# Attention and two MLPs on one core: the sums of the pooled softmax taken earlier on VectorE, and some splitting work moved to GpSimd

## The reference

```python
q_d, k_d, v_d = (a.reshape(B, H, S // 4, 4, D).mean(axis=3) for a in (q, k, v))
out_up = repeat(softmax(q_d @ k_d.T / 8) @ v_d, 4)            # pooled, 144 x 144
out_local = softmax(where(|i - j| < 4, q @ k.T / 8, -1e9)) @ v  # a band of 7
x = (out_up + out_local) laid out as (2304, 512)
x = ((x @ w1) * (x @ w2)) @ w3 @ w_out                        # d_ff 1024
out = silu(x @ w_in) @ w_out2                                 # d_ff 2048
```

## Time and profile before

| | us |
|---|---|
| median of 3 runs (lowest, highest) | 807.54 (807.38, 809.4) |
| the profiled execution | 807.54 |
| its span in the trace | 805.8 |
| PE busy | 790.7 (98%) |
| DVE busy | 597.3 (74%) |
| ACT busy | 347.7 (43%) |
| POOL busy | 267.3 (33%) |

### The profile page before, as it was taken

The page is one execution under the profiler, slowest core; times in us unless marked ns, Lnnn a source line. Parts: engine busy times, 40 slices in busy tenths (PEclk is TensorE's granted clock), DMA queues, the critical chain, the costliest instruction groups (busy, mean ns, idle before and its releaser), DMA issues.

```text
span 805.8 us, 13920 instructions
## 1 busy us (share of the span) xinstructions
PE 790.7 (98%) x5401; PEld 713.1 (88%) x5401; DVE 597.3 (74%) x952; ACT 347.7 (43%) x791; POOL 267.3 (33%) x341
## 2 busy tenths in 40 slices
PE   7999999999999999999999999999999999999998
PEld 6778888899998999999999898898889889888987
DVE  6998995767687676777678676779677679857644
ACT  6878877422344324432354333254223334433321
POOL 7788765422322331332213131113123113212100
PEclk9999999999999999999999999999999999999999
DMA  9857632110111111011121211223231122413102
GB/s 323 267 162 247 203 124 82 53 53 29 51 53 30 50 52 53 28 53 53 29 100 60 96 58 53 78 80 114 69 93 65 53 75 72 142 53 87 45 0 79
DMA packets 23041, 69.84 MB, mean 87 GB/s; under 512 B 2496, under 2 KB 2496, under 8 KB 22976
## 3 DMA queue, kind: packets, MB, share of 16 engines
q1 hardware_dynamic: 22976, 68.95, 26.3%
HBM read 64.23 MB, written 4.72 MB: 86 GB/s over the span
## 4 chain that ended last, share of the span: by engine, by line
PE 87%; DVE 9%; issue 1%; ACT 1%; DMA 1%; POOL 1%; SPq 0%; DVEq 0%; ACTq 0%; POOLq 0%
PE ps L1035 43%; PE ps L1093 25%; PE ps L1064 13%; PE ps L1115 3%; DVE qkd L741 1%; DVE prob L752 1%; DVE low L760 1%; DVE r L810 1%; DVE tr L704 1%; PE ps L1190 1%; DMA vg<-in_vg 1%; DVE lowd L766 1%; DVE w3t L733 1%; DVE x L795 1%; PE ps L1176 1%
## 5 line engine op out<-in xcount | busy, mean ns | idle before, releaser
L1035 PE MATMUL ps<-xb,wa 128*128 128x384 f32 x2016 | 405.2, 338 | 0.5 <-DVE mu L863 0.5
L1035 PEld LDWEIGHTS ps<-xb,wa 128*128 128x128 f32 x2016 | 355.1, 188 | 22.8 <-DVE mu L863 1.5
L380 POOL TENSOR_TENSOR rw<-rw 128x256 f32<-128x256 f32 x192 | 169.0, 901 | 451.0 <-DMA rw<-in_sets 337.6
L863 DVE TENSOR_TENSOR mu<-ps,mu 128x384 f32<-128x384 f32 x132 | 73.2, 555 | 121.2 <-PE ps L1035 120.4
L1064 PE MATMUL ps<-g,r 128*128 128x512 f32 (+1 forms) x576 | 124.9, 338 | 1.9 <-issue 1.9
L604 ACT ACTIVATE a<-a 128x384 f32<-128x384 f32 x72 | 37.9, 526 | 188.3 <-DVE a L863 188.3
L1093 PE MATMUL ps<-w2h_even,g 128*128 128x512 f32 x432 | 113.2, 394 | 0.0
L1093 PE MATMUL ps<-w2h_odd,g 128*128 128x512 f32 x432 | 112.5, 393 | 0.0
L710 DVE TENSOR_TENSOR wa<-rw,wa 128x1024 fp32r<-128x1024 f32 x96 | 106.8, 1113 | 3.6 <-ACT wa L443 3.5
L1064 PEld LDWEIGHTS ps<-g,r 128*128 128x128 f32 x576 | 97.7, 188 | 10.5 <-issue 2.5
L1093 PEld LDWEIGHTS ps<-w2h_odd,g 128*128 128x128 f32 x432 | 79.9, 188 | 11.9
(11 more groups left out here) (79 smaller groups left out, 727.5 us busy)
## 6 DMA issues: line engine op xcount, KB each, us to landing
rw<-in_sets SPq DMA_DIRECT2D x48, 512.0 KB, 3.5
w2r<-in_w_out SPq DMA_DIRECT2D x24, 512.0 KB, 3.5
qk<-in_qk SPq DMA_DIRECT2D x16, 576.0 KB, 6.6
vg<-in_vg SPq DMA_DIRECT2D x16, 336.0 KB, 4.3
vw<-in_vw SPq DMA_DIRECT2D x16, 320.0 KB, 3.2
out<-osb SPq DMA_DIRECT2D x18, 256.0 KB, 2.3
wn<-in_w SPq DMA_DIRECT2D x16, 256.0 KB, 4.5
raw<-in_w_out SPq DMA_DIRECT2D x2, 1024.0 KB, 12.3
```

The source lines that it names most:

```text
L380: nc.gpsimd.tensor_tensor(blocks[:, o, :], blocks[:, a, :], blocks[:, b, :], op).then_inc(done, 1)
L863: nc.vector.tensor_tensor(o, half_bank(k, i), term, ALU.add).then_inc(sum_ready, 1)
L1035: e = nc.tensor.matmul(ps[:, (k + i) % 2, 0:TH], wa[:, k % 2, l, A_SLOT[i], a * P:(a + 1) * P], xb[:, i, r, a, :], start=(i in (0, 1, 4) a ...
```

## The change

It is confined to the attention part:

- DVE: `totals_down(s)`, which stood behind `min_local(s+1)`, now stands behind `w3_low`, ahead of the low parts of `w_out`, of `EXTRA`, and of `mask_local(s+1)` and `min_local(s+1)`. In step 0 `min_local(1)` comes right behind `totals_local(0)`. The low parts of `w_out` move from behind `max_down` to behind `totals_down`.
- `W_OUT` is spread over three steps instead of four (three, three, two blocks), and the middle block of each (1, 4, 7) gets its low part on GpSimd, at the head of its step; there are two semaphores instead of one, and PE waits for the one that belongs to the block.
- ACT: `copy_ptd` moves from ahead of `exps_down` to behind it. The factor 1/4 of the pooled values goes from `take_down` into `totals_down`.
- The sums: 1e-9 is added by a `tensor_scalar` instruction instead of by a reduction over pairs whose second element GpSimd had filled with 1e-9.
- GpSimd: `norm_d` ahead of `shift_local(s+1)` except in step 0, and the second set of weight sums in steps 9 to 12 instead of behind step 15.
- Loads: `qk(1)` is issued by ACT at its start; SP's first ones are qk(0), vg(0), vw(0), qk(2); the first half of `w_out` goes behind qk(3) and vg(2).
- Eight warm-up transposes instead of nine.

```diff
-        W_OUT = {1: (0, 1), 2: (2, 3), 3: (4, 5), 4: (6, 7)}
+        W_OUT = {1: (0, 1, 2), 2: (3, 4, 5), 3: (6, 7)}
+        R3_POOL = [W_OUT[s][1] for s in W_OUT]
...
@@ SP @@
-            for s in range(3):
-                load_qk(s)
-                if s == 1:
-                    load_vg(0)
-                    load_vw(0)
+            load_qk(0)
+            load_vg(0)
+            load_vw(0)
+            load_qk(2)
             for t in range(PAIRS):
                 if t == 1:
-                    load_w_out(0)
                     load_qk(3)
                 if t + 1 < PAIRS:
                     load_vg(t + 1)
+                if t == 1:
+                    load_w_out(0)
...
@@ GpSimd, step @@
+                for n in W_OUT.get(s - 1, ())[1:2]:
+                    pool.wait_ge(r3_hi, n + 1)
+                    nc.gpsimd.tensor_tensor(r3[:, n, 1, :], raw3[:, n, BANK:], r3[:, n, 0, :].bitcast(F32),
+                                            ALU.subtract).then_inc(r3_lo_pool, 1)
                 pool_values()
                 if s == 0:
                     shift_local(0)
-                if SUMS[0] <= s < SUMS[0] + 4:
-                    weight_sum(0, s - SUMS[0])
+                for k in range(2):
+                    if SUMS[k] <= s < SUMS[k] + 4:
+                        weight_sum(k, s - SUMS[k])
                 pool.wait_ge(inv_l, s + 1)
                 nc.gpsimd.tensor_tensor(pr, pr, inv[:, u, :, None].broadcast_to([P, 10, BW]), ALU.mult
                                         ).then_inc(norm_l, 1)
-                if s + 1 < PAIRS:
+                if s == 0:
+                    shift_local(1)
+                pool.wait_ge(inv_d, s + 1)
...
+                if 0 < s < PAIRS - 1:
                     shift_local(s + 1)
-                normalise_down()
...
@@ ACT @@
+            act.dma_start(qk_at(1).rearrange("p c s -> p (c s)"), qk_in[1, :, :]).then_inc(qk_here[1], 16)
...
-                    nc.scalar.activation(od[:, (s - 1) % 2, :], ps[:, pO, 0:SD], ACT.Copy, scale=1.0 / POOL
-                                         ).then_inc(od_ready, 1)
+                    copy_act(od[:, (s - 1) % 2, :], ps[:, pO, 0:SD]).then_inc(od_ready, 1)
...
                 if s > 0:
                     copy_pt()
-                    copy_ptd()
                 if s == 0:
                     act.wait_ge(blank, 2)
                 exps_down()
+                if s > 0:
+                    copy_ptd()
...
@@ DVE @@
-                nc.vector.tensor_reduce(tot1[:, u, :], tot[:, u, :, :], AX.X, ALU.add).then_inc(added_l, 1)
+                nc.vector.tensor_scalar(tot1[:, u, :], tot[:, u, :], 1e-9, None, ALU.add).then_inc(added_l, 1)
...
-                nc.vector.tensor_reduce(totd1[:, u, :], totd[:, u, :, :], AX.X, ALU.add).then_inc(added_d, 1)
+                nc.vector.tensor_scalar(totd1[:, u, :], totd[:, u, :], 1e-9, float(POOL), ALU.add,
+                                        ALU.mult).then_inc(added_d, 1)
...
                 max_down(s)
-                for n in W_OUT.get(s - 1, ()):
-                    dve.wait_ge(r3_hi, n + 1)
-                    nc.vector.tensor_tensor(r3[:, n, 1, :], raw3[:, n, BANK:], r3[:, n, 0, :].bitcast(F32),
-                                            ALU.subtract).then_inc(r3_lo, 1)
                 if s == 0:
                     mask_local(1)
                 elif s + 1 < PAIRS:
                     pool_pair(s + 1)
                 totals_local(s)
+                if s == 0:
+                    min_local(1)
                 for q in splits_of(s):
                     w3_low(q)
+                totals_down(s)
+                for n in W_OUT.get(s - 1, ())[0::2]:
+                    dve.wait_ge(r3_hi, n + 1)
+                    nc.vector.tensor_tensor(r3[:, n, 1, :], raw3[:, n, BANK:], r3[:, n, 0, :].bitcast(F32),
+                                            ALU.subtract).then_inc(r3_lo_dve, 1)
                 if s in EXTRA:
...
                 if 0 < s < PAIRS - 1:
                     mask_local(s + 1)
-                if s < PAIRS - 1:
                     min_local(s + 1)
-                totals_down(s)
...
@@ PE @@
-                    pe.wait_ge(r3_lo, n + 1)
+                    if n in R3_POOL:
+                        pe.wait_ge(r3_lo_pool, R3_POOL.index(n) + 1)
+                    else:
+                        pe.wait_ge(r3_lo_dve, n - sum(m < n for m in R3_POOL) + 1)
...
-            warm(9)
+            warm(8)
```

More of the change, by code:

```diff
@@ L141, in attention_then_mlps @@
         gate = sb("gate", [1, 2])
-        tot = sb("tot", [P, 2, 10, 2])
-        totd = sb("totd", [PD, 2, 4, 2])
+        tot = sb("tot", [P, 2, 10])
+        totd = sb("totd", [PD, 2, 4])
         tot1 = sb("tot1", [P, 2, 10])
@@ L149, in attention_then_mlps @@
         vt = sb("vt", [KC, 3, 2 * D])
-        sb("hold2", [P, 1024 - 80 - 42 - 28 - 6 * D])
+        sb("hold2", [P, 1024 - 80 - 42 - 6 * D])
         ps = ctx.enter_context(nc.psum_tensor("ps", [P, 8, BANK], F32))
@@ L165, in attention_then_mlps @@
         consts = sem("consts")
-        blank, small = sem("blank"), sem("small")
+        blank = sem("blank")
         scored, p_turned, summed_d, summed_l = sem("scored"), sem("p_turned"), sem("summed_d"), sem("summed_l")
@@ L180, in attention_then_mlps @@
             sem("w3_hi"), sem("w3_lo"), sem("w3_mul"), sem("w3o_hi"), sem("w3o_lo"))
-        r3_hi, r3_lo = sem("r3_hi"), sem("r3_lo")
+        r3_hi, r3_lo_dve, r3_lo_pool = sem("r3_hi"), sem("r3_lo_dve"), sem("r3_lo_pool")
         tr_ready, xb_hi, xb_lo = sem("tr_ready"), sem("xb_hi"), [sem(f"xb_lo{n}") for n in range(7)]
@@ L205, in attention_then_mlps @@
         LATE = 3
-        W_OUT = {1: (0, 1), 2: (2, 3), 3: (4, 5), 4: (6, 7)}
+        W_OUT = {1: (0, 1, 2), 2: (3, 4, 5), 3: (6, 7)}
+        R3_POOL = [W_OUT[s][1] for s in W_OUT]
         SUMS = (5, 9)
         HIGHS = (7, 9)
-        EXTRA = {9: ("weights", 0), 10: ("tokens", 0), 11: ("tokens", 1), 12: ("tokens", 2), 13: ("tokens", 3),
-                 14: ("weights", 1)}
         FILL = {1: (30, 4, 2), 2: (6, 6, 2), 3: (6, 6, 2)}
@@ L422, in step @@
                                         ).then_inc(norm_l, 1)
-                if s + 1 < PAIRS:
+                if s == 0:
+                    shift_local(1)
+                pool.wait_ge(inv_d, s + 1)
+                pd = prob_d[:, u, :, :, 0:SD].rearrange("p c h k -> p (c h) k")
+                nc.gpsimd.tensor_tensor(pd, pd, invd[:, u, :, None].broadcast_to([PD, 4, SD]), ALU.mult
+                                        ).then_inc(norm_d, 1)
+                if 0 < s < PAIRS - 1:
                     shift_local(s + 1)
-                normalise_down()
             for s in range(PAIRS):
                 step(s)
-            for i in range(4):
-                weight_sum(1, i)
             pool.wait_ge(xb_hi, 3)
@@ L496, in exps_down @@
                                                      scale=D ** -0.5 / POOL ** 2,
-                                                     accum_out=totd[:, u, 2 * g + h, 0:1])
+                                                     accum_out=totd[:, u, 2 * g + h:2 * g + h + 1])
                     e.then_inc(exp_d, 1)
@@ L505, in exps_local @@
                             e = nc.scalar.activation(pr, pr, ACT.Exp, bias=low[:, u, n:n + 1], scale=-1.0,
-                                                     accum_out=tot[:, u, n, 0:1])
+                                                     accum_out=tot[:, u, n:n + 1])
                     e.then_inc(exp_l, 1)
@@ L772, in totals_local @@
                 dve.wait_ge(exp_s, s + 1)
-                nc.vector.tensor_reduce(tot[:, u, 2 * LATE:10, 0].rearrange("p (g h) -> p g h", h=2),
+                nc.vector.tensor_reduce(tot[:, u, 2 * LATE:10].rearrange("p (g h) -> p g h", h=2),
                                         prob[:, u, LATE:NG, :, :], AX.X, ALU.add).then_inc(sum_l, 1)
@@ L839, in _ @@
             pool_pair(0)
-            dve.wait_ge(small, 2)
             mask_local(0)
```

2 lines of the change are left out of this document (removed).

## The result

| | before | after |
|---|---|---|
| median, us (runs) | 807.46 (4) | 818.75 (4) |
| lowest, highest | 807.34, 809.4 | 818.4, 820.48 |
| profiled execution | 807.54 | 818.61 |
| its span | 805.8 | 816.8 |

The ratio is 1.0139, with a 95% interval of 1.0117 to 1.016: 11.3 us slower, where 8.1 had been forecast (815.6, range 811 to 820). The sign, the mechanism and the range held; the size was 3 us short, and two mis-sized terms partly hid each other.

What follows compares the result with a forecast made beforehand. DVE was taken as full in steps 3 to 5, PE and DVE in later steps. +3.4 us by step 3's start and 4.7 from there to step 15 made +8.1 on 807.5: 815.6 us, range 811 to 820.

Steps and rivals of the forecast that it cites:

- The ring by DVE: Attention steps: DVE waits for ACT's pooled exponentials before the next step's minimum, which ACT awaits; 7.35 + X us per step.
- exp_d(3): End of ACT's exponentials of the pooled scores in step 3 (one pair of heads), forecast at 35.15 us.
- The small instructions behind the wait: Two small DVE instructions after the wait for pooled exponentials, 0.16 each: 0.33 us with the signal.
- X: DVE work placed between `totals_down` and the next mask: 1.0 us in steps 10 to 14, 1.7 per pair of low parts.
- The ring by PE: Attention steps: PE's `weighted_down` waits for the late `copy_ptd`; 7.8 us per step against 7.57.
- The start: Loads and steps 0 to 2: qk(0) lands at 5.9 us, sharing with qk(1); +3.4 us by step 3's start on ACT.
- A(2): Moment ACT begins the exponentials of step 2, forecast 21.4 us against 19.16; A(3), A(15) likewise for steps 3, 15.
- The end: From ACT's start of step 15 to the first MLP product, 21.3 us: same work, nothing given back.
- PE's clock: Rival, 4%: PE's clock falls in new gaps of 0.3 to 1.8 us; at worst over 825 us.
- The rival on the other side: Rival, 5%: the freed DVE wins, attention steps shrink to PE's 7.57 us; 804.5 at best, 806 with half.
- Slack that I do not see: Rival, 17%: early copies and qk(0) cost nothing, only late steps pay: 810 to 812.5 us.
- GpSimd gets in first: Rival, 12%: GpSimd's `norm_d` starts before DVE's token sum, 2.0 us in five steps, +5: 820 us.

Runs made afterwards that it cites:

- the run with the reduction: The changed kernel with the reduction over pairs holding 1e-9 instead of `tensor_scalar`, factor 1/4 back in `take_down`: 818.23 us, ratio 1.013.
- the version above: Kernel before plus w_out low parts split two, three, three (one each on GpSimd), second weight sums in steps 9 to 12, later w_out load: 805.51 us.
- the one with the moved sums alone: The kernel before with only `totals_down(s)` moved directly behind `w3_low`: 817.19 us, ratio 1.0122.
- the one with fillers: The changed kernel with 8, 12 and 16 more warm-up transposes on PE in steps 1, 2 and 3, ahead of `weighted_down`: 819.83 us, ratio 1.0148.
- the kernel of the experiment on the start: The changed kernel with qk(1) as SP's second load again, nothing on ACT's queue: median 819.34 us, ratio 1.0147.

## Why the prediction held, and where it was short

- **The ring by DVE.** Right, and right in its parts: 5.25 us on ACT (5.25 measured), 1.77 for mask and minimum (1.77), DVE idle ahead of the wait 15 times. Alone in the kernel before it costs 9.9 us. From exp_d(3) to exp_d(14) it is 90.74 us, where 90.25 had been added up.
- **The small instructions behind the wait, 0.33 us.** Mis-sized: I carried 0.15 over from a reduction to a `tensor_scalar`, bounded it by 0.05, and it took 0.46 on average, up to 1.23, because it ended only with GpSimd's multiplication.
- **X.** Too large: 0.84 to 0.9 for 768 elements against 1.0, and about 1.2 for a pair of low parts against 1.7. These errors have the opposite sign to the last one and the same source: DVE waits for GpSimd, and I had the right collision at the wrong instruction, as the run with the reduction shows, where the pair took 2.4. That the step came within 0.1 us of its 8.35 is in part luck.
- **The ring by PE.** Right: counted from exp_d to exp_d, the passes without extra work took 7.80 or 7.81 us (forecast 7.8), and the late copy alone costs 5.4 us.
- **The start.** +3.9 against +3.4. qk(0) came at 6.39, at the late end of the bound; I took 5.9, and two equal loads side by side should have been put near the late end. The Trainium skill, "DMA: Bandwidth & Descriptors", section "Queues, rings and completion order", says that a DMA engine takes turns between queues packet by packet; the landing at 6.39 agrees with what the prediction made of it. ACT's three copies and the waiting take_down put A(2) at 21.83 (21.4 forecast).
- **The end.** The step that failed: "Nothing given back", priced at 0. It cost 0.9. PE's weighted_down(14) waits for the late copy until 135.33 and pushes its products back behind both of its parts, 2.24 us, to 137.57; before, it had been done with that. In the earlier trace rows and in the experiments whose clock held here, the way from A(15) to the first MLP product is 22.2 to 22.3 us in every kernel with the late copy and 21.3 to 21.4 in every kernel with the early one, so the late copy is the cause. The ring was followed for 14 steps and not out of the last.
- **PE's clock**, a rival of 4%: it fell once in the profiled execution of the changed kernel, at 36 us, and cost nothing there. Where it fell in other kernels and the step had to wait for PE, it cost 0.8 to 1.5 us. The reason I gave against it, that it had been 1.00 in all stretches before, was weak: that kernel has one gap of this size, 1.79 us at 13.01, and one gap without a fall says little of the next.
- **The rival on the other side** (804.5 to 806) was wrong for this change and right for a part of it: 805.51 in the version above.
- **The other two rivals.** "Slack that I do not see" put nothing on the early steps; A(3) is 3.9 us later. "GpSimd gets in first" needed token sums of 2.0 us; behind invd they took 0.93 to 0.95.
- **The range.** The bounds listed for it add up to 812.4 and 822.0 around 815.6, and not to the 811 and 820 that were stated. 818.75 lies within either.

## What to carry to other kernels

When an instruction with a wait is moved up in a queue, look for what now stands behind it and whether that feeds, through other engines, the very thing it waits for: a wait off the path becomes a ring, and its length is the sum of rows that the old trace already shows. Two such rings side by side cost about the longer one, so undo suspects one by one and together. And price every instruction that changes its kind by a row of the new kind, however small it is: what it computes is nothing, what it may have to wait for is not.

## What the runs showed of the hardware

A `tensor_scalar` of 72 x 4 float32 elements on DVE took between 0.17 and 1.23 us in the changed kernel. In 14 of 16 cases a GpSimd multiplication was running, and the instruction ended within 0.04 us of it; the reduction in its place took 0.14 to 0.16 in all 16 steps. Of two loads of 576 KB issued at the same time (0.74 us) on two queues, the first landed 1.84 us later than with both on one queue. PE's granted clock fell to the lower level behind some of the idle times of 1.6 to 2.2 us at PE (0.58 in 36 to 39 of the changed kernel, 0.53 in 105 to 108 of the one with the moved sums alone, 0.60 in 138 to 141 of the one with fillers) and not behind others as long (2.14 us in the kernel of the experiment on the start, 1.84 in the one with the moved sums alone, clock 1.00).
